# Order of the second network's first projection and the first network's third pair, and of two ScalarE steps

## The chip, the cores and the metric

The kernel runs on one core of a Trainium2 chip. The metric is the device time of one execution in microseconds. Its five engines run streams of their own: TensorE (PE; its weight loads are shown apart as PEld), VectorE (DVE), ScalarE (ACT), GpSimd (POOL) and SyncE (SP), which starts the DMA transfers here. They meet only through semaphores.

## The reference, cut to what matters

```python
kv_pool = kv.reshape(B, H // 4, 4, W // 4, 4, C).mean(axis=(2, 4))
k = v = kv_pool.reshape(B, -1, C) @ w_sr             # 768 keys, C = 128
s = (q @ k.transpose(0, 2, 1)) / np.sqrt(C)          # 12288 tokens
a = np.exp(s - s.max(-1, keepdims=True))
a /= a.sum(-1, keepdims=True) + 1e-09
x = (a @ v).reshape(-1, C)
h = x @ w_in                                         # first network, 128 -> 2048
x = (h * (1.0 / (1.0 + np.exp(-1.702 * h)))) @ w_out # 2048 -> 128
h = x @ w_in2                                        # second network
return (h * np.clip(h + 3.0, 0.0, 6.0) / 6.0) @ w_out2
```

## The kernel before, in words

The 12288 tokens are worked through in NT = 24 tiles of 512. Everything that TensorE multiplies is split into a high part (rounded to the format fp32r) and a low part (what is left), and each product is three matmuls: high by high, low weights by high data, high weights by low data. `product` (L1080 on) issues them, so nearly all matmuls of the profile have the lines L1082, L1083 and L1086.

A network's 2048 hidden features are handled as 8 pairs of 128-feature chunks (PAIRS = 8). For pair p of tile t:

- `hidden1(t, p)` and `hidden2(t, p)` (TensorE, 6 matmuls of 512 columns) compute the pair's hidden values of the first and the second network into PSUM. In the loop hidden1 always uses the tile pair[2], and waits for the gelu before it (`act1_ready`); hidden2 uses pair[0] and pair[1] in turn.
- First network: `gelu` (ScalarE, L589) takes PSUM to `work`, `act1_hi` (ScalarE, L604) rounds it to `mid_hi`, `act1_lo` (VectorE, L891) subtracts to `mid_lo`.
- Second network: `gate` (ScalarE, L616), `hard_swish` (VectorE, L904), `act2_hi` (ScalarE, L628) and `act2_lo` (VectorE, L912) do the same.
- `project1(t, p)` and `project2(t, p)` (TensorE, 6 matmuls each) multiply by the output weights and add up over the pairs in the PSUM banks `bank_av` and `bank_out`.

One loop turn i works on four tiles at once: the first network of tile i, the second network of tile i - 1, the attention scores of tile i + 2 and the weighing of values of tile i + 1. The order of every engine is written out by hand; there is no planner. Turn 1 has an order of its own, turns 2 to 21 are a hardware loop, turns 22 and 23 are written out with the same function and leave out the attention work for which no tile is left.

On TensorE, `job(i, j)` is hidden1(i, j/2) for even j and hidden2(i - 1, j/2 rounded down) for odd j; `finish_job(i, j)` is project1(i, ·) or project2(i - 1, ·) in the same way. A turn begins hidden2(i - 1, 0), hidden1(i, 0), project2(i - 2, 7), hidden2(i - 1, 1), hidden1(i, 1), project1(i, 0). Then j runs on from 4, each step followed by the projection three steps behind it (LAG = 3): hidden1(i, 2), project2(i - 1, 0), hidden2(i - 1, 2), project1(i, 1), and so on. After the last comes `between`: the scores for tile i + 2 and the weighing for tile i + 1.

The accumulator `bank_out` is used by one tile after another. So `project2` with p = 0 waits until the previous tile's result has been transposed out of it (`turn_y`, VectorE, L929, 128x512 to `y_sb`):

```python
pe.wait_ge(mid2_hi_ready, PAIRS * t + p + 1)      # L1383
if p == 0 and later(t) and output2_in(t) is bank_out:
    pe.wait_ge(y_ready, t)
```

At the start of a turn VectorE does, in this order: `scale_x` (L853), the inverse of the sums, `x1_low` (L862), the transposition of one tile's probabilities in four slots (`turn_p`, L836), of which the first three stand ahead of hard_swish 0 and the fourth behind it, then act1_lo 0, act2_lo 0, turn_y, hard_swish 1, act1_lo 1, `turn_q` (L804), act2_lo 1, act1_lo 2, hard_swish 2. ScalarE does gate 0, gelu 0, act1_hi 0, act2_hi 0, gelu 1, gate 1, act1_hi 1, gelu 2, act2_hi 1, act1_hi 2, gate 2, and then for each further pair gelu, act2_hi of the pair before, act1_hi, gate. An engine's instructions start strictly in order, so one that waits holds all behind it.

Of the kernel before, what the change touches and what calls it, by code (L numbers as in the profile page):

```python
# [12 lines left out]
def attention_and_two_ffns(nc, q, kv, w_sr, w_in1, w_out1, w_in2, w_out2, out):  # L13
# [17 lines left out]
    PAIRS = FC // 2  # L31
# [21 lines left out]
    with ExitStack() as ctx:  # L53
# [69 lines left out]
        def mid2(t, p):  # L123
            return (p + 2) % 4 if isinstance(t, int) and t == NT - 1 else 2 + p % 2
# [60 lines left out]
        def hidden1_in(t, p):  # L185
            return pair[(2, 1, 0)[p % 3]] if isinstance(t, int) and t == 0 else pair[2]
# [5 lines left out]
        def activated1(t, p):  # L192

            return hidden1_in(t, p)[:, :] if isinstance(t, int) and t == 0 else act1[p % 2]
# [115 lines left out]
        def of_pair(c):  # L310
            return slice(0, PAIR) if c is None else slice(c * TILE, (c + 1) * TILE)
# [4 lines left out]
        def in_pair(data, t, p, c):  # L316

            if c is not None and isinstance(t, int) and t == NT - 1 and p == PAIRS - 1:
                return data[:, :].rearrange("p (c n) -> p c n", c=2)[:, :, of_tile(c)]
            return data[:, of_pair(c)]  # L320
# [7 lines left out]
        def later(value):  # L328
            return not isinstance(value, int) or value > 0
# [173 lines left out]
        def _(act):  # L503
# [16 lines left out]
            def q_high(u):  # L520
                act.wait_ge(qt_ready, u - 1)
                if isinstance(u, int) and u == 2:
                    act.wait_ge(scores_ready, SLOTS)
                else:
                    act.wait_ge(scores_ready, SLOTS * u)
                act.activation(q_hi[:, :], q_t[:, :], ACT.Copy, scale=SCALE).then_inc(q_hi_ready, 1)
# [21 lines left out]
            def p_hi(t, n):  # L548
                act.wait_ge(p_landed, 16 * 16 * t)
                cols = slice(n * PAIR, (n + 1) * PAIR)  # L550
                act.activation(p_high[:, cols], p_keys[:, cols], ACT.Copy).then_inc(p_hi_ready, 1)
# [28 lines left out]
            def gelu(t, p, c=None):  # L580
                n = PAIRS * t + p
                part = of_pair(c)
                if c == 0:
                    act.wait_ge(h1_half_ready, 1)
                else:
                    act.wait_ge(h1_ready, n + 1)
                if later(t):
                    act.wait_ge(mid1_ready, n - 1)
                act.activation(activated1(t, p)[:, part], hidden1_in(t, p)[:, part],  # L589
                               ACT.Gelu_apprx_sigmoid).then_inc(act1_half_ready if c == 0 else act1_ready, 1)  # L590

            def act1_hi(t, p, c=None):
                n = PAIRS * t + p
                part = of_pair(c)
                if c == 0 and p == 0:
                    act.wait_ge(act1_half_ready, 1)
                else:
                    act.wait_ge(act1_ready, n + 1)
                if isinstance(t, int) and t == 0:
                    if p > 3:  # L600
                        act.wait_ge(out1_done, p - 3)
                else:
                    act.wait_ge(out1_done, n - 1)
                act.activation(mid_hi[mid1(t, p)][:, part], activated1(t, p)[:, part],  # L604
                               ACT.Copy).then_inc(mid1_half_hi_ready if c == 0 else mid1_hi_ready, 1)

            def gate(t, p, c=None):
                n = PAIRS * t + p
                first_half = p == 0 and c == 0
                if first_half:  # L610
                    act.wait_ge(h2_half_ready, 1)
                else:
                    act.wait_ge(h2_ready, n + 1 + (c if c and p else 0))
                if later(n - 1) and not c:
                    act.wait_ge(act2_ready, n - 1)
                act.activation(in_pair(gate2[p % 2], t, p, c), hidden_part(t, p, c), ACT.Relu,  # L616
                               bias=half[:, :], scale=1.0 / 6.0).then_inc(gate2_half_ready if first_half else gate2_ready, 1)

            def act2_hi(t, p, c=None):
                n = PAIRS * t + p  # L620
                act.wait_ge(act2_ready, n + 1 + (c or 0))
                if isinstance(t, int) and t == NT - 1 and p in (2, 3):
                    act.wait_ge(out1_done, PAIRS * NT)
                elif isinstance(t, int) and t == NT - 1 and p > 3:
                    act.wait_ge(out2_done, n - 3)
                elif later(n - 1):
                    act.wait_ge(out2_done, n - 1)
                act.activation(in_pair(mid_hi[mid2(t, p)], t, p, c), in_pair(act2[p % 2], t, p, c),  # L628
                               ACT.Copy).then_inc(mid2_hi_ready, 1)
# [7 lines left out]
            def load_table(func):  # L637
                act.activation(warm[:, :], half[:, :], func)
# [69 lines left out]
            def iteration(i, with_q=True, with_p=True, scored=True, begun=0, late=0):  # L708
                for p in range(begun, PAIRS):
                    if p == 0:  # L710
                        gate(i - 1, p)
                    if p == 1:
                        act2_hi(i - 1, p - 1)
                    gelu(i, p)
                    if p == 1:
                        gate(i - 1, p)
                    if 1 < p < PAIRS - 1:
                        act2_hi(i - 1, p - 1)
                    act1_hi(i, p)
                    if p == PAIRS - 1:  # L720
                        act2_hi(i - 1, p - 1)
                    if p > 1:
                        gate(i - 1, p)
                    if p == 3 + late and with_q:
                        q_high(i + 2)
                    if 4 + late <= p < 4 + late + P_PARTS and with_p:
                        p_hi(i + 1, p - 4 - late)
                if scored:
                    load_table(ACT.Exp)
                x2_high(i)  # L730
                act2_hi(i - 1, PAIRS - 1)
                if scored:
                    for s in range(SLOTS):
                        exponential(i + 2, s)
                if with_p:
                    x1_high(i + 1)
                if scored:
                    load_table(ACT.Gelu_apprx_sigmoid)

            iteration(1, begun=4, late=1)  # L740
            with act.Fori(2, NT - 2) as i:
                iteration(i)
# [336 lines left out]
        def _(pe):  # L1079
# [309 lines left out]
            def job(i, j):  # L1389
                if j % 2 == 0:  # L1390
                    hidden1(i, j // 2)
                else:
                    hidden2(i - 1, j // 2)

            def finish_job(i, j):
                if j % 2 == 0:
                    project1(i, j // 2)
                else:
                    project2(i - 1, j // 2)
# [49 lines left out]
            def iteration(i, scored_too=True, weighed=True):  # L1449

                if later(i - 1):
                    job(i, 1)
                    job(i, 0)
                    finish_job(i - 1, JOBS - 1)

                    job(i, 3)
                    job(i, 2)
                    finish_job(i, 0)
                    begun = 4
                else:  # L1460
                    hidden2(0, 0)
                    hidden2(0, 1)
                    hidden1(1, 0)
                    hidden2(0, 2)
                    hidden2(0, 3)
                    project2(0, 0)
                    hidden1(1, 1)
                    project1(1, 0)
                    hidden1(1, 2)
                    project2(0, 1)  # L1470
                    project1(1, 1)
                    hidden1(1, 3)
                    project1(1, 2)

                    project2(0, 2)
                    hidden1(1, 4)
                    begun = 9
                for j in range(begun, JOBS):
                    job(i, j)
                    if j >= LAG:  # L1480
                        finish_job(i, j - LAG)
                finish_job(i, JOBS - 2)
                if scored_too:
                    between(i)
                elif weighed:
                    for k in range(KC):
                        weigh(i + 1, k)
                finish_job(i, JOBS - 3)
# [38 lines left out]
```

## Time and profile before

| | us |
|---|---|
| median of three runs | 1280.79 (1280.19 to 1281.34) |
| the profiled execution's own time | 1280.32 |
| its span in the profile | 1278.6 |
| TensorE busy | 1270.0 (5800 matmuls) |
| VectorE busy | 1034.1 |
| ScalarE busy | 1027.4 |
| GpSimd busy | 34.4 |

The span runs from the first to the last instruction that the profiler saw; the time of the execution has 1.7 us more around it. Busy shares tell which engine could be the bound, the view of waits who stood still for whom, and a timeline of a short window in which order things end. In a timeline row the first number is the start and the second the duration. A matmul's duration overlaps its successor's, so a rate is read from the distances between starts. A weight load of an undelayed matmul starts together with the matmul before it. The profile numbers lines by kernel.py.

### The profile page before, as it was taken

To read this page: it belongs to the slowest core of one execution; us is meant where nothing else is said; L and a number is where in the kernel's file an instruction comes from. 1 tells how busy PE (TensorE), PEld (TensorE's weight loads), DVE (VectorE), ACT (ScalarE), POOL (GpSimd) and SP (SyncE) were. 2 spreads that over 40 slices of the span, in tenths; PEclk is the share of its full clock that TensorE was granted. 3 is DMA by queue.
4 is the path that set the end of the run, shared out by engine and by line. 5 is a ranking of instruction groups with operands and counts; after the bars stand their busy time and mean duration, and the time that the engine had idled before them with its cause. 6 is when DMAs were issued, how large, how long until landed. Compare 5 with 4: busy or idle time off the path is not lost.

```text
span 1278.6 us, 18310 instructions
## 1 busy us (share of the span) xinstructions
PE 1270.0 (99%) x5800; PEld 1055.4 (83%) x5800; DVE 1034.1 (81%) x1084; ACT 1027.4 (80%) x1216; POOL 34.4 (3%) x46
## 2 busy tenths in 40 slices
PE   8999999999999999999999999999999999999998
PEld 7888888888888888888888888888888888888887
DVE  5788887888878878888788888887888878887768
ACT  3888877888788888887788878888888778887776
POOL 1800000000000000000000000000000000000000
PEclk9999999999999999999999999999999999999999
DMA  8421321303213123032130220311303213022001
GB/s 280 126 44 40 75 46 28 74 9 65 57 17 74 30 44 74 0 74 49 25 74 13 60 63 11 74 34 40 74 0 74 49 25 74 18 47 67 1 9 17
DMA packets 183685, 65.69 MB, mean 51 GB/s; under 512 B 104560, under 2 KB 176368, under 8 KB 183408
## 3 DMA queue, kind: packets, MB, share of 16 engines
q1 hardware_dynamic: 182576, 65.30, 22.3%
q10 hardware_dynamic: 1088, 0.13, 0.1%
q8 instruction: 11, 0.18, 0.1%
q14 instruction: 10, 0.08, 0.0%
HBM read 22.87 MB, written 6.34 MB: 23 GB/s over the span
## 4 chain that ended last, share of the span: by engine, by line
PE 97%; SPq 1%; DMA 1%; DVE 0%; ACT 0%; issue 0%; DVEq 0%
PE pair L1082 14%; PE pair L1083 14%; PE pair L1086 14%; PE bank_av L1082 9%; PE bank_av L1083 9%; PE bank_av L1086 9%; PE bank_out L1086 7%; PE bank_out L1083 7%; PE bank_out L1082 7%; PE score_banks L1086 2%; PE score_banks L1083 2%; PE score_banks L1082 2%; DMA kv_sb<-in_kv_dram 1%; SPq L354 0%; SPq L362 0%; SPq L366 0%
## 5 line engine op out<-in xcount | busy, mean ns | idle before, releaser
L912 DVE TENSOR_TENSOR mid_lo<-work,mid_hi 128x1024 fp32r<-128x1024 f32 (+1 forms) x193 | 233.9, 1212 | 112.5 <-ACT mid_hi L628 112.4
L1082 PE MATMUL pair<-x_hi,w_hi 128*128 128x512 f32 (+1 forms) x774 | 300.7, 388 | 0.0
L1083 PE MATMUL pair<-x_hi,w_lo 128*128 128x512 f32 (+1 forms) x774 | 300.0, 388 | 0.0
L1086 PE MATMUL pair<-x_lo,w_hi 128*128 128x512 f32 (+1 forms) x774 | 299.9, 387 | 0.0
L589 ACT ACTIVATE work<-pair 128x1024 f32<-128x1024 f32 x184 | 189.2, 1028 | 120.8 <-PE pair L1086 118.5
L904 DVE SCALAR_TENSOR_TENSOR work<-work,pair 128x1024 f32<-128x1024 f32 (+1 forms) x194 | 232.9, 1201 | 15.3 <-ACT work L616 14.6
L891 DVE TENSOR_TENSOR mid_lo<-work,mid_hi 128x1024 fp32r<-128x1024 f32 x184 | 223.6, 1215 | 25.1 <-ACT mid_hi L604 25.0
L616 ACT ACTIVATE work<-pair,half 128x1024 f32<-128x1024 f32 (+1 forms) x194 | 213.1, 1099 | 4.3 <-PE pair L1086 4.2
L628 ACT ACTIVATE mid_hi<-work 128x1024 fp32r<-128x1024 f32 (+1 forms) x193 | 201.8, 1046 | 2.3 <-DVE work L904 2.3
L604 ACT ACTIVATE mid_hi<-work 128x1024 fp32r<-128x1024 f32 x184 | 194.7, 1058 | 1.6
L1082 PEld LDWEIGHTS pair<-x_hi,w_hi 128*128 128x128 f32 x774 | 145.3, 188 | 33.7 <-ACT work L589 4.2
L1086 PEld LDWEIGHTS pair<-x_lo,w_hi 128*128 128x128 f32 x774 | 145.4, 188 | 29.8
L1083 PEld LDWEIGHTS pair<-x_hi,w_lo 128*128 128x128 f32 x774 | 145.4, 188 | 28.8
L1086 PE MATMUL bank_av<-mid_lo,w_hi 128*128 128x512 f32 x398 | 154.9, 389 | 0.0
L1082 PE MATMUL bank_av<-mid_hi,w_hi 128*128 128x512 f32 x398 | 154.9, 389 | 0.0
L1083 PE MATMUL bank_av<-mid_hi,w_lo 128*128 128x512 f32 x398 | 154.8, 389 | 0.0
L1086 PE MATMUL bank_out<-mid_lo,w_hi 128*128 128x512 f32 x368 | 143.2, 389 | 0.0
L1082 PE MATMUL bank_out<-mid_hi,w_hi 128*128 128x512 f32 x368 | 143.2, 389 | 0.0
L1083 PE MATMUL bank_out<-mid_hi,w_lo 128*128 128x512 f32 x368 | 143.2, 389 | 0.0
L541 ACT ACTIVATE probs<-score_banks,neg_max 128x768 f32<-128x768 f32 x88 | 78.1, 900 | 80.8 <-DVE neg_max L813 80.8
L813 DVE TENSOR_REDUCE neg_max<-score_banks 128x1 f32<-128x768 f32 x88 | 78.3, 950 | 42.6 <-PE score_banks L1086 42.6
L1086 PEld LDWEIGHTS bank_av<-mid_lo,w_hi 128*128 128x128 f32 x398 | 74.7, 188 | 15.7 <-DVE mid_lo L891 0.2
(175 smaller groups left out, 1560.2 us busy)
## 6 DMA issues: line engine op xcount, KB each, us to landing
p_keys<-p_turned SPq DMA_DIRECT2D x368, 96.0 KB, 2.2
inv_b<-inv_dram SPq DMA_DIRECT2D x23, 256.0 KB, 3.2
out_dram<-y_sb SPq DMA_DIRECT2D x92, 64.0 KB, 2.4
q_raw<-in_q_dram SPq DMA_DIRECT2D x88, 64.0 KB, 2.0
kv_sb<-in_kv_dram SPq DMA_DIRECT2D x6, 768.0 KB, 9.4
w_raw<-in_moe_w_in_dram SPq DMA_DIRECT2D x2, 1024.0 KB, 8.0
kv_sb<-in_kv_dram SPq DMA_DIRECT2D x6, 256.0 KB, 8.1
inv_dram<-inv_t SPq DMA_DIRECT2D x92, 0.5 KB
```

The source lines that it names most:

```text
L541: act.activation(two(slot(dst, s)), scored_slot(u, s), ACT.Exp, bias=neg_max[:, s:s + 1], accum_out=p_sum[:, s:s + 1]).then_inc(exp_ready, 1)
L589: act.activation(activated1(t, p)[:, part], hidden1_in(t, p)[:, part], ACT.Gelu_apprx_sigmoid).then_inc(act1_half_ready if c == 0 else act ...
L604: act.activation(mid_hi[mid1(t, p)][:, part], activated1(t, p)[:, part], ACT.Copy).then_inc(mid1_half_hi_ready if c == 0 else mid1_hi_read ...
L616: act.activation(in_pair(gate2[p % 2], t, p, c), hidden_part(t, p, c), ACT.Relu, bias=half[:, :], scale=1.0 / 6.0).then_inc(gate2_half_rea ...
L628: act.activation(in_pair(mid_hi[mid2(t, p)], t, p, c), in_pair(act2[p % 2], t, p, c), ACT.Copy).then_inc(mid2_hi_ready, 1)
L813: dve.reduce_max(neg_max[:, s:s + 1], scored_slot(u, s), AX_XY, negate=True).then_inc(max_ready, 1)
L891: dve.tensor_tensor(mid_lo[mid1(t, p)][:, part], activated1(t, p)[:, part], mid_hi[mid1(t, p)][:, part], ALU.subtract).then_inc(mid1_half_ ...
L904: last = dve.scalar_tensor_tensor(out=in_pair(act2[p % 2], t, p, c), in0=in_pair(gate2[p % 2], t, p, c), scalar=1.0, in1=hidden_part(t, p, c),
L912: dve.tensor_tensor(in_pair(mid_lo[mid2(t, p)], t, p, c), in_pair(act2[p % 2], t, p, c), in_pair(mid_hi[mid2(t, p)], t, p, c), ALU.subtrac ...
L1082: pe.matmul(dst, a_hi, b_hi, start=start, stop=False)
L1083: pe.matmul(dst, a_lo, b_hi, start=False, stop=False)
L1086: return pe.matmul(dst, a_hi, b_lo, start=False, stop=stop)
```

## The change

On TensorE, in turns 2 to 23, project2(i - 1, 0) is issued ahead of hidden1(i, 2) instead of behind it: the turn begins hidden2 0, hidden1 0, project2(i - 2, 7), hidden2 1, hidden1 1, project1 0, project2 0, hidden1 2, and then goes on as before with hidden2 2, project1 1. On ScalarE, in the same turns, act2_hi 1 is issued ahead of gelu 2 instead of behind it. Turn 1, whose pairs below 4 are written out apart on ScalarE, isn't touched. The number of instructions, their shapes, the buffers and the conditions they wait for are the same.

```diff
--- before.py
+++ after.py
@@ -711,10 +711,12 @@
                         gate(i - 1, p)
                     if p == 1:
                         act2_hi(i - 1, p - 1)
+                    if p == 2:
+                        act2_hi(i - 1, p - 1)
                     gelu(i, p)
                     if p == 1:
                         gate(i - 1, p)
-                    if 1 < p < PAIRS - 1:
+                    if 2 < p < PAIRS - 1:
                         act2_hi(i - 1, p - 1)
                     act1_hi(i, p)
                     if p == PAIRS - 1:
@@ -1456,7 +1458,9 @@
                     job(i, 3)
                     job(i, 2)
                     finish_job(i, 0)
-                    begun = 4
+                    finish_job(i, 1)
+                    job(i, 4)
+                    begun = 5
                 else:
                     hidden2(0, 0)
                     hidden2(0, 1)
```

## Rows read from the trace of the kernel before

**Rows 1.** The page: TensorE busy, and its granted clock in slices.
```profile
PE 1270.0 (99%) x5800; PEld 1055.4 (83%) x5800; DVE 1034.1 (81%) x1084; ACT 1027.4 (80%) x1216; POOL 34.4 (3%) x46
...
PEclk9999999999999999999999999999999999999999
```

**Rows 2.** Waits; who waited for whom: us in total, times, longest us.
```profile
PEld pair L1082 <- ACT work L589: 4.2, 23, 0.2
```

**Rows 3.** Busy time of each engine in two windows (x instructions).
```profile
532.90:584.72 51.82, 51.82 (x236) 43.03 (x235) 42.54 (x45) 42.59 (x50) 0.00 (x0) 1.00 0.21 46
...
588.72:598.27 9.55, 9.55 (x44) 7.81 (x43) 9.34 (x13) 8.30 (x11) 0.00 (x0) 1.00 0.11 25
```

**Rows 4.** Timeline, TensorE, turn 11: start, duration in us, [idle before <- releaser].
```profile
597.42 0.39 PE L1083 MATMUL bank_av<-mid_hi,w_lo 128*128 128x512 f32 x1
...
597.65 0.39 PE L1086 MATMUL bank_av<-mid_lo,w_hi 128*128 128x512 f32 x1
597.79 0.19 PEld L1082 LDWEIGHTS pair<-x_hi,w_hi 128*128 128x128 f32 x1 [0.18 <-ACT work L589]
...
599.29 0.39 PE L1082 MATMUL bank_out<-mid_hi,w_hi 128*128 128x512 f32 x1
```

**Rows 5.** Timeline, VectorE, the same turn, and the instructions of line 929.
```profile
588.72 0.69 DVE L853 TENSOR_TENSOR x_full<-bank_av,inv_b 128x512 f32<-128x512 f32 x1 [0.30 <-PE bank_av L1086]
...
596.43 1.21 DVE L912 TENSOR_TENSOR mid_lo<-work,mid_hi 128x1024 fp32r<-128x1024 f32 x1
597.56 0.71 DVE L929 STREAM_TRANSPOSE y_sb<-bank_out 128x512 f32<-128x512 f32 x1
598.78 1.22 DVE L904 SCALAR_TENSOR_TENSOR work<-work,pair 128x1024 f32<-128x1024 f32 x1 [0.51 <-ACT work L616]
...
L929 DVE STREAM_TRANSPOSE y_sb<-bank_out x23: 708/711/718, 131.0 to 1253.9; 128x512 f32<-128x512 f32 x23
```

**Rows 6.** Timeline, ScalarE, the same turn.
```profile
594.74 1.04 ACT L628 ACTIVATE mid_hi<-work 128x1024 fp32r<-128x1024 f32 x1
596.71 1.03 ACT L589 ACTIVATE work<-pair 128x1024 f32<-128x1024 f32 x1 [0.93 <-PE pair L1086]
...
599.58 1.02 ACT L589 ACTIVATE work<-pair 128x1024 f32<-128x1024 f32 x1
...
604.93 1.03 ACT L589 ACTIVATE work<-pair 128x1024 f32<-128x1024 f32 x1 [1.43 <-PE pair L1086]
```

**Rows 7.** Timeline, turn 2 and turn 23.
```profile
131.02 0.71 DVE L929 STREAM_TRANSPOSE y_sb<-bank_out 128x512 f32<-128x512 f32 x1
...
131.27 0.39 PE L1086 MATMUL bank_av<-mid_lo,w_hi 128*128 128x512 f32 x1
...
1214.74 0.71 DVE L929 STREAM_TRANSPOSE y_sb<-bank_out 128x512 f32<-128x512 f32 x1
...
1215.33 0.39 PE L1086 MATMUL bank_av<-mid_lo,w_hi 128*128 128x512 f32 x1
...
1215.81 0.40 PE L1083 MATMUL pair<-x_hi,w_lo 128*128 128x512 f32 x1
```

**Rows 8.** Timeline, before the loop: a load behind VectorE.
```profile
20.30 0.68 DVE L798 SCALAR_TENSOR_TENSOR q_lo<-bank_out,q_hi 128x512 fp32r<-128x512 f32 x1
...
21.10 0.19 PEld L1082 LDWEIGHTS pair<-k_hi,q_hi 128*128 128x128 f32 x1
```

**Rows 9.** Timeline, before the loop: a late load and the matmuls around it.
```profile
73.63 0.39 PE L1086 MATMUL pair<-x_lo,w_hi 128*128 128x512 f32 x1
...
73.98 0.19 PEld L1082 LDWEIGHTS pair<-x_hi,w_hi 128*128 128x128 f32 x1 [0.39 <-ACT probs L541]
...
75.96 0.39 PE L1086 MATMUL pair<-x_lo,w_hi 128*128 128x512 f32 x1
```

**Rows 10.** Timeline, TensorE, the first microseconds: eight like matmuls, twice.
```profile
2.92 4.18 PE L1170 MATMUL pair<-patch,ident 128*128 128x288 f32 x8 [2.92 <-POOL ident L463]
...
8.62 2.14 PE L1170 MATMUL pair<-patch,ident 128*128 128x288 f32 x8
```

## The prediction

> **What bounds the kernel now.** I read the page's busy shares first. TensorE is busy 1270.0 of 1278.6 us, at the full granted clock (2.4 GHz of its two levels) in all 40 slices [rows 1]. So the time is TensorE's instruction stream plus whatever holds it up, and any new gap in that stream is paid in full.
>
> Next comes the view of waits, kept to TensorE's weight loads, since that is where a stalled matmul shows. One wait belongs to the loop: 23 times, 0.2 us at most, 4.2 us in all, on ScalarE's gelu, L589 [rows 2]. Then the busy times in a window of one loop turn: 51.82 us long, TensorE busy for all of it, while VectorE and ScalarE work 42.5 us each [rows 3]. With so little to take away, I went to the timeline of the place that the diff touches, first TensorE [rows 4], then VectorE [rows 5] and ScalarE [rows 6].
>
> **What can be gained.** hidden1(i, 2) must wait until gelu 1 has emptied the one PSUM pair that all of hidden1 uses. gelu 1 runs from 596.71 to 597.74 [rows 6]. The weight load follows at 597.79, where an undelayed one starts together with the matmul before it, at 597.65 [rows 4]. That is 0.14 us late, but loads run ahead of matmuls, so little of it is lost. The undelayed distance between 128x512 matmuls is 0.227 us (597.42 to 597.65). From 597.65 to 599.29 lie seven of them, 1.59 us undelayed, and they took 1.64. So the turn loses 0.05 us; turn 23 loses 0.04 (1215.33 to 1215.81, two distances, 0.48 against 0.45 at least; the rest follows) [rows 7]. The change sends six matmuls, project2(i - 1, 0), ahead, 6 x 0.227 = 1.36 us, and gelu 1 is then done long before. The wait goes in the 22 turns i = 2 to 23 that take the changed branch: 22 x 0.04 = 0.9 us. The 23rd is in turn 1, whose order is written out apart and stays. This is all that there is to gain, 0.07%.
>
> **What the moved step meets.** project2(i - 1, 0) issues six matmuls and no DMA, but it has three conditions: the high half of pair 0, its low half, and y_ready at L1384, because it opens a new sum in bank_out and VectorE must first have transposed the previous tile's result out of that bank (turn_y, L929). Today it starts at 599.29, when all three are met. Moved, its first weight load is due at 597.65 and its first matmul 0.227 after that. The high half is ready: rounding ends at 594.74 + 1.04 = 595.78 [rows 6]. The low half ends at 596.43 + 1.21 = 597.64, and the third matmul, whose load is due near 598.10, needs it; no loss. But turn_y runs from 597.56 to 598.27 [rows 5]. It is 0.62 us too late for a load due at 597.65.
>
> Could VectorE be earlier? Its work there hangs on TensorE itself: scale_x starts at 588.72 after an idle 0.30 that ends with TensorE's weighing, and in the 9.55 us from there to the end of turn_y VectorE is busy 9.34 us in 13 instructions [rows 3, 5]. Nothing that TensorE does in between is reordered before project1(i, 0) ends, and VectorE's order is untouched. So the 0.62 us stays in every turn and cannot heal by itself: if TensorE stalls, the next turn's scores come later and VectorE's chain with them.
>
> **The cost of one stall.** The load starts some time after turn_y ends. Lower bound 0.05 us, as after gelu 1 (597.74 to 597.79) [rows 4, 6]. Upper bound 0.12, from a place where TensorE also stands behind several waits in line: q_lo ends at 20.98, the load starts at 21.10 [rows 8]. The delay of the load is thus 0.67 to 0.74; since project2 has two waits ahead of its first matmul, I take 0.72. Not all of the load's delay is lost. At 73.98 a load came 0.35 us after its due time 73.63; from 73.63 to 75.96 lie nine distances, 2.04 undelayed, and they took 2.33: 0.29 lost, 0.06 less than the delay [rows 9]. At 597.79 it was 0.09 less. So a stall costs 0.58 to 0.68; I take 0.64.
>
> It isn't the same in all turns. Turn_y stands 23 times in the trace, of 708 to 718 ns [rows 5]; turns 3 to 22, twenty of them, look like the one shown. In turn 2 it ends at 131.73 against a due time of 131.27, 0.46 late: 0.46 + 0.10 - 0.08 = 0.48. In turn 23 no probabilities are turned any more; it ends at 1215.45 against 1215.33: 0.12 + 0.10 - 0.08 = 0.14 [rows 7].
>
> **What else moves.** Behind the waiting matmul stand, in TensorE's strict order, hidden1(i, 2), hidden2(i - 1, 2) and project1(i, 1). hidden1(i, 2) now starts 1.36 + 0.64 = 2.0 us later than before and gelu 2, which started at 599.58 with its input just complete, can't start before about 601.4. Here ScalarE's reordering matters: act2_hi 1 waits for hard_swish 1, which ends at 598.78 + 1.22 = 600.00 [rows 5], so it runs 600.05 to 601.10 in time that ScalarE would now idle, and gelu 2 follows at 601.4 undelayed, ending at 602.4. hidden1(i, 3) has its load due at about 603.7 (project2, hidden1, hidden2 and project1, 24 matmuls or 5.44 us, after 598.5, less one distance), 1.3 us of slack. The edit of ScalarE's order costs nothing; were gelu 2 left ahead of it, act2_hi 1 would start near 602.3, and it too is only needed by project2(i - 1, 1) some 3 us later. From pair 3 on the order is the old one, and ScalarE waits for TensorE there (1.43 us before the gelu at 604.93 [rows 6]), so nothing else becomes late. No DMA queue is passed.
>
> **The sum.** Against the profiled execution's own 1280.32 us (span 1278.6, 1.7 around it): 20 x 0.64 = 12.8, + 0.48 + 0.14 = 13.4, - 0.9 regained = + 12.5, so 1292.8. That execution lay 0.5 us below the median 1280.79 of the runs shown; with half of that I predict 1293.0 us, slower by 0.95%. By the bounds, 20 x 0.58 + 0.6 - 0.9 = + 11.3 and 20 x 0.68 + 0.6 - 0.9 = + 13.3.
>
> **Rivals.**
> Rival A, the wait is hidden (not slower). Mechanism: turn_y's end falls before the load's due time, so only the old stall goes: 1280.8 - 0.9 = 1279.9. It decides from the point at which VectorE's stretch from 588.72 to 598.27 is 0.62 us shorter. Turn 23 speaks for it, where the transposes of probabilities are gone; the lateness is 0.12 [rows 7]; but twenty turns carry them, and nothing in the change removes any. A gain over 0.2%, 2.6 us, would need three times the whole loss that exists.
>
> Rival B, a second wait: gelu 2, behind act2_hi 1, becomes late for hidden1(i, 3). The 1.3 us of slack would have to be used up; a further 0.3 us a turn gives 1293 + 22 x 0.3 = 1299.6. The idle rows of ScalarE speak against it.
>
> Rival C, the clock: a gap in each turn makes TensorE fall to the lower of its levels for a while. The first eight 288-column matmuls of the trace took 4.18 us, eight later ones 2.14 [rows 10], so a matmul may double. If only the twelve after the gap did, 12 x 0.227 = 2.7 us a turn, 22 x 2.7 = 60 us, 1353. Against it: after the 0.39 us gap at 73.98 the distances were back at 0.227 within five matmuls [rows 9]. The clock row shows no dip in any slice [rows 1], but it reads 9 in the first slice too, which holds the slow eight, so the distances are the better witness. The Trainium skill, "TensorE: Matmul & The Clock Gate", section "A second HAM failure mode: psum-queue depth-cycling", says that small gaps between matmul groups, one per cycle of a PSUM queue, can make the clock swing; by that rule rival C holds, and the trace so far disagrees, with gaps half as long.
>
> **Chances.** Forecast 0.90, A 0.04, B 0.03, C 0.01; the last 0.02 for a gain by something that I don't see. About 0.2% is what a measurement of this kernel can tell from no change. So slower 0.94, same 0.04, faster 0.02. The range holds the forecast with its bounds (1291.6 to 1294.1 by the runs' median), widened for the spread of runs and a mis-sized restart to 1290.0 to 1295.5.
>
> **What would show it.** Right: in the waits, the gelu entry shrinks from 23 to one or two, and a new one, bank_out's weight loads behind VectorE's L929, stands some 22 times with 0.6 to 0.7 us each, about 14 us. A turn is 52.4 instead of 51.82 us. Wrong: no idle before bank_out in turn 3 to 22 (rival A), idle before pair's loads behind L589 later in the turn (B), or distances of 0.4 us after the gap (C). The forecast falls if turn_y isn't what releases project2, or if its end is earlier against TensorE than 0.6 us after the due time.

## The result, and the profile after

The changed kernel takes 1292.57 us (median of five runs, 1292.35 to 1293.27) against 1280.79: ratio 1.0094, 95% interval 1.0083 to 1.0106. The forecast was 1293.0 us, with a range of 1290.0 to 1295.5. The profiled execution took 1292.57 us, its span 1290.8. In kernel.py the lines behind the ScalarE edit stand two further down: L1082, L1083 and L1086 are now L1084, L1085 and L1088, L912 is L914, turn_y's L929 is L931.

The page first, busy times and granted clock. The clock is as in [rows 1]. The number of matmuls is the same, and the weight loads' busy time too (1055.0 us against 1055.4). "PE busy" rose by 4 us, not by 12: the modelled duration of a matmul overlaps its successor's and covers a part of each gap.

```profile
PE 1274.1 (99%) x5800; PEld 1055.0 (82%) x5800; DVE 1036.2 (80%) x1084; ACT 1035.4 (80%) x1216; POOL 34.5 (3%) x46
...
PEclk9999999999999999999999999999999999999999
```

The waits. Of the 23 waits on the gelu in [rows 2] one is left, that of turn 1; new are 22 loads of bank_out that stood idle for 16.3 us in all. Of each idle (0.77 us in most turns), some 0.04 us are the ordinary space between two loads, so the delay is 0.73.

```profile
PEld bank_out L1084 <- issue: 16.3, 22, 0.8
...
PE bank_out L1084 <- DVE y_sb L931: 7.7, 21, 0.4
...
PEld pair L1084 <- ACT work L589: 0.2, 1, 0.2
```

These two rows are the same event. The load's row says "issue" and the matmul's row names turn_y, with less than half of the time. The wait for y_ready is an instruction of its own in TensorE's queue ahead of the load, so nothing on the load itself names a releaser. The views leave this instruction out, but the trace holds it: in turn 11 a semaphore instruction of L1386 stands from 603.34 to 603.39, just ahead of the load at 603.41.

A loop turn (columns as in [rows 3]: length, then PE, PEld, DVE, ACT busy). It is 52.42 us long, 0.60 more than in [rows 3], and for 0.38 us of it TensorE isn't busy.

```profile
551.18:603.60 52.42, 52.04 (x235) 43.01 (x235) 42.63 (x44) 42.94 (x51) 0.00 (x0) 1.00 0.21 45
```

The place of the change in turn 11, as in [rows 4] and [rows 5]: start, duration, and idle with its releaser.

```profile
602.45 0.39 PE L1085 MATMUL bank_av<-mid_hi,w_lo 128*128 128x512 f32 x1
...
602.59 0.71 DVE L931 STREAM_TRANSPOSE y_sb<-bank_out 128x512 f32<-128x512 f32 x1
...
602.68 0.39 PE L1088 MATMUL bank_av<-mid_lo,w_hi 128*128 128x512 f32 x1
603.41 0.19 PEld L1084 LDWEIGHTS bank_out<-mid_hi,w_hi 128*128 128x128 f32 x1 [0.77 <-issue]
603.45 0.47 PE L1084 MATMUL bank_out<-mid_hi,w_hi 128*128 128x512 f32 x1 [0.38 <-DVE y_sb L931]
...
603.75 0.40 PE L1085 MATMUL bank_out<-mid_hi,w_lo 128*128 128x512 f32 x1
...
604.22 0.40 PE L1084 MATMUL bank_out<-mid_hi,w_hi 128*128 128x512 f32 x1
```

The last matmul of project1(i, 0) starts at 602.68, and bank_out's first load is due with it. turn_y ends at 602.59 + 0.71 = 603.30 and the load starts at 603.41. From 602.68 to 604.22 lie four distances (the matmul between 603.75 and 604.22 isn't shown), 0.91 us undelayed, and they took 1.54: 0.63 lost. The turns say the same: 51.82 us before, with 0.04 lost to the gelu, and 52.42 now, so the stall costs 0.60 + 0.04 = 0.64 us.

Turn 2 and turn 23, in answer to [rows 7]: loads due at 131.03 and 1227.45 start at 131.60 and 1227.69.

```profile
130.78 0.71 DVE L931 STREAM_TRANSPOSE y_sb<-bank_out 128x512 f32<-128x512 f32 x1
...
131.03 0.39 PE L1088 MATMUL bank_av<-mid_lo,w_hi 128*128 128x512 f32 x1
131.60 0.19 PEld L1084 LDWEIGHTS bank_out<-mid_hi,w_hi 128*128 128x128 f32 x1 [0.60 <-issue]
...
1226.86 0.71 DVE L931 STREAM_TRANSPOSE y_sb<-bank_out 128x512 f32<-128x512 f32 x1
...
1227.45 0.39 PE L1088 MATMUL bank_av<-mid_lo,w_hi 128*128 128x512 f32 x1
...
1227.69 0.19 PEld L1084 LDWEIGHTS bank_out<-mid_hi,w_hi 128*128 128x128 f32 x1 [0.28 <-issue]
```

ScalarE after the gap: act2_hi 1 ends at 606.12, gelu 2 waits for TensorE until 606.47.

```profile
605.06 1.06 ACT L628 ACTIVATE mid_hi<-work 128x1024 fp32r<-128x1024 f32 x1 [0.34 <-DVE work L906]
606.47 1.03 ACT L589 ACTIVATE work<-pair 128x1024 f32<-128x1024 f32 x1 [0.34 <-PE pair L1088]
```

### The profile page after: what moved, and what is told of

It is laid out like the page before. It is cut to its first block, busy times and chain, and to the rows that moved or that the text cites. A ratio compares the mean times of both kernels' runs of the same rounds, so it can differ in the third digit from the quotient of the medians.

```text
span 1290.8 us, 18310 instructions
## 1 busy us (share of the span) xinstructions
PE 1274.1 (99%) x5800; PEld 1055.0 (82%) x5800; DVE 1036.2 (80%) x1084; ACT 1035.4 (80%) x1216; POOL 34.5 (3%) x46
## 4 chain that ended last, share of the span: by engine, by line
PE 82%; DVE 11%; issue 4%; ACT 1%; DVEq 1%; DMA 1%; SPq 0%
PE pair L1084 11%; PE pair L1088 11%; PE pair L1085 11%; PE bank_av L1088 9%; PE bank_av L1084 9%; PE bank_av L1085 9%; PE bank_out L1084 5%; PE bank_out L1088 5%; PE bank_out L1085 5%; DVE p_turned L838 3%; PE score_banks L1088 2%; PE score_banks L1085 2%; PE score_banks L1084 2%; DVE mid_lo L914 2%; DVE work L906 2%
## 5 line engine op out<-in xcount | busy, mean ns | idle before, releaser
L914 DVE TENSOR_TENSOR mid_lo<-work,mid_hi 128x1024 fp32r<-128x1024 f32 (+1 forms) x193 | 233.8, 1212 | 106.8 <-ACT mid_hi L628 106.7
L1084 PE MATMUL pair<-x_hi,w_hi 128*128 128x512 f32 (+1 forms) x774 | 300.2, 388 | 0.0
L1088 PE MATMUL pair<-x_lo,w_hi 128*128 128x512 f32 (+1 forms) x774 | 299.9, 387 | 0.0
L1085 PE MATMUL pair<-x_hi,w_lo 128*128 128x512 f32 (+1 forms) x774 | 299.8, 387 | 0.0
L628 ACT ACTIVATE mid_hi<-work 128x1024 fp32r<-128x1024 f32 (+1 forms) x193 | 201.6, 1045 | 9.8 <-DVE work L906 9.8
L1084 PEld LDWEIGHTS pair<-x_hi,w_hi 128*128 128x128 f32 x774 | 145.3, 188 | 30.4 <-ACT probs L541 0.4
L1088 PEld LDWEIGHTS pair<-x_lo,w_hi 128*128 128x128 f32 x774 | 145.4, 188 | 29.8
L1085 PEld LDWEIGHTS pair<-x_hi,w_lo 128*128 128x128 f32 x774 | 145.3, 188 | 29.7
L1088 PE MATMUL bank_av<-mid_lo,w_hi 128*128 128x512 f32 x398 | 154.9, 389 | 0.0
L1084 PE MATMUL bank_av<-mid_hi,w_hi 128*128 128x512 f32 x398 | 154.9, 389 | 0.0
L1085 PE MATMUL bank_av<-mid_hi,w_lo 128*128 128x512 f32 x398 | 154.9, 389 | 0.0
L1084 PE MATMUL bank_out<-mid_hi,w_hi 128*128 128x512 f32 x368 | 145.0, 394 | 7.7 <-DVE y_sb L931 7.7
L1088 PE MATMUL bank_out<-mid_lo,w_hi 128*128 128x512 f32 x368 | 143.3, 389 | 0.0
L1085 PE MATMUL bank_out<-mid_hi,w_lo 128*128 128x512 f32 x368 | 143.3, 389 | 0.0
L1084 PEld LDWEIGHTS bank_out<-mid_hi,w_hi 128*128 128x128 f32 x368 | 69.0, 188 | 29.8 <-issue 16.3
```

The lines of the kernel that those rows point to most:

```text
L914: dve.tensor_tensor(in_pair(mid_lo[mid2(t, p)], t, p, c), in_pair(act2[p % 2], t, p, c), in_pair(mid_hi[mid2(t, p)], t, p, c), ALU.subtrac ...
L1084: pe.matmul(dst, a_hi, b_hi, start=start, stop=False)
L1085: pe.matmul(dst, a_lo, b_hi, start=False, stop=False)
L1088: return pe.matmul(dst, a_hi, b_lo, start=False, stop=stop)
```

## The experiments

All times are medians of 4 to 11 runs; the kernel before took 1280.5 to 1280.7 us beside them. "Ratio" is against the kernel before, with its 95% interval.

### ScalarE's half alone

```diff
 # against the changed kernel, TensorE
-                    finish_job(i, 1)
-                    job(i, 4)
-                    begun = 5
+                    begun = 4
```

> Only ScalarE's half of the change: act2_hi 1 ahead of gelu 2, TensorE in the old order. My theory: ScalarE's order costs nothing. act2_hi 1 starts when hard_swish 1 has ended (600.00 in the trace of before), gelu 2 follows at 601.1 instead of 599.6 and ends at 602.1, a microsecond ahead of the load of hidden1(i, 3), due at 603.15. So 1280.8 us, within 0.3 of before. Rival (part of the loss comes from ScalarE): if gelu 2 became late for hidden1(i, 3), this kernel would be slower than before, by up to the whole 11.8 us.

Measured: 1280.74 us, ratio 0.9999 (0.9990 to 1.0008). The gelu's entry in the waits is that of before, and in the timeline gelu 2 follows act2_hi 1 (548.74, L628) at 549.71 and ends at 550.71, 1.13 us ahead of the load of hidden1(i, 3) at 551.84. The waits:

```profile
PEld pair L1084 <- ACT work L589: 4.2, 23, 0.2
```

The timeline of ScalarE in turn 10:

```profile
548.74 1.06 ACT L628 ACTIVATE mid_hi<-work 128x1024 fp32r<-128x1024 f32 x1 [0.34 <-DVE work L906]
549.71 1.00 ACT L589 ACTIVATE work<-pair 128x1024 f32<-128x1024 f32 x1
```

ScalarE's edit has no part in the loss.

### TensorE's half alone

```diff
 # against the changed kernel, ScalarE
-                    if p == 2:
-                        act2_hi(i - 1, p - 1)
                     gelu(i, p)
...
-                    if 2 < p < PAIRS - 1:
+                    if 1 < p < PAIRS - 1:
                         act2_hi(i - 1, p - 1)
```

> Only TensorE's half: project2(i - 1, 0) ahead of hidden1(i, 2), ScalarE in the old order with gelu 2 ahead of act2_hi 1. My theory: the whole loss is here, 1292.6 us, within 0.3 of the changed kernel, with the same 0.77 us idle ahead of bank_out's first weight load in every turn. Rival: if the rounding step ahead of gelu 2 were what costs, this kernel would be back near 1280; if on the contrary it saved something, this one would be slower than 1292.6.

Measured: 1292.86 us, ratio 1.0094 (1.0079 to 1.0110), with the changed kernel's two rows of waits to the tenth. ScalarE now idles 1.72 us before gelu 2 and rounds pair 1 behind it. VectorE's act2_lo 1 waits for that, 1.66 us in the turn shown, but no load of TensorE gets a new wait from it. The whole loss is in TensorE's order. The waits:

```profile
PEld bank_out L1082 <- issue: 16.3, 22, 0.8
...
PE bank_out L1082 <- DVE y_sb L929: 7.7, 21, 0.4
```

The timeline of ScalarE and VectorE in turn 10:

```profile
555.07 1.03 ACT L589 ACTIVATE work<-pair 128x1024 f32<-128x1024 f32 x1 [1.72 <-PE pair L1086]
555.99 1.05 ACT L628 ACTIVATE mid_hi<-work 128x1024 fp32r<-128x1024 f32 x1
...
557.07 1.23 DVE L912 TENSOR_TENSOR mid_lo<-work,mid_hi 128x1024 fp32r<-128x1024 f32 x1 [1.66 <-ACT mid_hi L628]
```

### turn_y made early: both waits gone

```diff
 # against the changed kernel, VectorE
-                    if p == 0 and with_p:
-                        turn_p(i + 1, 3)
                     if p == 1:
                         hard_swish(i - 1, p)
...
                     if p == 0:
-                        act2_lo(i - 1, p)
                         turn_y(i - 2)
+                        act2_lo(i - 1, p)
+                    if p == 0 and with_p:
+                        turn_p(i + 1, 3)
```

> The changed kernel, and VectorE's turn_y moved up: the fourth turn_p of a turn goes from ahead of act1_lo 0 to behind act2_lo 0, and turn_y goes ahead of act2_lo 0. My theory (the wait on turn_y is all of the loss): act1_lo 0 then runs 594.9 to 596.1 on the old scale, turn_y 596.0 to 596.7, act2_lo 0 to 597.85; loads due at 597.65 and 598.10, so neither wait is late, nor is gelu 1's. Expected 1279.9 us, 0.9 under before. Rival (any reordering of project2 and hidden1 costs some 0.6 us a turn by itself, through the PSUM banks or the weight loads): stays near 1292.6. Rival (turn_p is too late for the transfers of the probabilities behind it): a new wait of ScalarE or TensorE on the weighing, 1285 or more.

Measured: 1279.40 us (eleven runs, 1279.15 to 1279.79), ratio 0.9990 (0.9981 to 0.9999). This is the fastest kernel of the study. In the rows: a turn is 51.78 us with TensorE busy throughout; turn_y ends at 544.94, 0.94 ahead of the load due at 545.88; act2_lo 0 ends at 546.05, and the loads follow each other at 0.227 us. turn_p (L838) now fills the place in which VectorE used to idle before hard_swish 1 (0.51 us in [rows 5]). The busy times in one turn:

```profile
532.57:584.35 51.78, 51.78 (x236) 43.10 (x235) 42.71 (x45) 42.82 (x50) 0.00 (x0) 1.00 0.21 46
```

The timeline of VectorE in turn 10:

```profile
544.23 0.71 DVE L931 STREAM_TRANSPOSE y_sb<-bank_out 128x512 f32<-128x512 f32 x1
544.87 1.18 DVE L914 TENSOR_TENSOR mid_lo<-work,mid_hi 128x1024 fp32r<-128x1024 f32 x1
545.97 0.97 DVE L838 STREAM_TRANSPOSE p_turned<-probs 128x768 f32<-128x768 f32 x1
547.00 1.22 DVE L906 SCALAR_TENSOR_TENSOR work<-work,pair 128x1024 f32<-128x1024 f32 x1
```

And of TensorE's weight loads:

```profile
545.88 0.19 PEld L1084 LDWEIGHTS bank_out<-mid_hi,w_hi 128*128 128x128 f32 x1
546.10 0.19 PEld L1085 LDWEIGHTS bank_out<-mid_hi,w_lo 128*128 128x128 f32 x1
546.33 0.19 PEld L1088 LDWEIGHTS bank_out<-mid_lo,w_hi 128*128 128x128 f32 x1
```

So moving project2(i - 1, 0) costs nothing by itself, and it wins back what the gelu's stall had cost, once the bank is free in time. By the times the gain is 1.3 us, and the interval leaves 0.1 to 2.4; the rows show 0.04 us a turn, 0.9 in 22. The rival of a fixed price per reordering falls, and so does that of late probabilities.

### VectorE's order alone, with TensorE as before

The same VectorE edit, on the kernel before.

> The kernel before, with VectorE's order of the experiment beside it (fourth turn_p behind act2_lo 0, turn_y ahead of act2_lo 0) and nothing else. My theory: VectorE's order is no gain in itself, since TensorE's only stall in the old order is gelu 1: 1280.8 us, within 0.3 of before, with the 0.18 us idle on L589 in 23 turns as before. Rival (VectorE's order helps TensorE by itself, for instance by sooner low halves): as fast as the experiment beside it, 1279.9 or less.

Measured: 1280.74 us, ratio 1.0002 (0.9993 to 1.0011). The gelu's wait stands as before:

```profile
PEld pair L1082 <- ACT work L589: 4.2, 23, 0.2
```

VectorE's order is worth nothing without the moved projection; the 1.3 us between this kernel and the one above, measured side by side, need both edits.

### How late turn_y is: a smaller lateness

```diff
 # against the changed kernel, VectorE
-                    if p == 0 and with_p:
-                        turn_p(i + 1, 3)
...
                     if p == 0:
                         act2_lo(i - 1, p)
                         turn_y(i - 2)
+                    if p == 0 and with_p:
+                        turn_p(i + 1, 3)
```

> The changed kernel, and on VectorE only the fourth turn_p of a turn moved from ahead of act1_lo 0 to behind turn_y. act1_lo 0 can't move up by the whole 0.88 us, since it needs act1_hi 0 (ends 594.83 on the old scale); turn_y then ends about 597.86 instead of 598.27. My theory (the loss is the lateness of turn_y's end, one for one): the load comes 0.32 us late instead of 0.73, a stall costs 0.24 instead of 0.64, 20 turns x 0.24 + 0.2 for turns 2 and 23 - 0.9 = + 4.1, so 1284.9 us. Rival (the loss is a fixed price of the moved step): 1292.6.

Measured: 1284.40 us, ratio 1.0030 (1.0019 to 1.0042). The load is 548.45 - 548.12 = 0.33 us late, as worked out. The waits:

```profile
PEld bank_out L1084 <- issue: 7.7, 22, 0.4
```

The timeline of turn 10:

```profile
547.62 0.71 DVE L931 STREAM_TRANSPOSE y_sb<-bank_out 128x512 f32<-128x512 f32 x1
...
548.12 0.39 PE L1088 MATMUL bank_av<-mid_lo,w_hi 128*128 128x512 f32 x1
...
548.45 0.19 PEld L1084 LDWEIGHTS bank_out<-mid_hi,w_hi 128*128 128x128 f32 x1 [0.36 <-issue]
```

### turn_y first: the next condition in line

```diff
 # against the changed kernel, VectorE
                     if p == 0:
-                        act2_lo(i - 1, p)
                         turn_y(i - 2)
+                        act2_lo(i - 1, p)
```

> The changed kernel, and on VectorE only turn_y and act2_lo 0 change places. turn_y ends at 597.14 on the old scale, in time; act2_lo 0 ends at 598.27, and the third matmul of project2(i - 1, 0), whose load is due at 598.10, needs it. My theory: the wait moves there, with a load 0.22 us late, some 0.13 lost a turn: 20 x 0.13 - 0.9 = + 1.7, so 1282.5 us, and the idle stands ahead of bank_out's load of line L1088 on VectorE's L914. Rival (project2's first matmul is held by something else than turn_y): 1292.6.

Measured: 1281.39 us, ratio 1.0007 (0.9997 to 1.0016), 1.1 less than expected. The wait moved to where it was expected, the third matmul's load (L1088) behind act2_lo 0 (L914), 21 times; the load is 546.64 - 546.45 = 0.19 us late. I had put 0.22: act2_lo 0 takes 1.18 us here, not 1.21. Against the kernel with neither wait, 2.0 us over 21 turns are 0.09 a turn instead of the 0.13 that I had allowed. The waits:

```profile
PEld bank_out L1088 <- DVE mid_lo L914: 4.7, 21, 0.2
```

The timeline of turn 10:

```profile
545.40 1.18 DVE L914 TENSOR_TENSOR mid_lo<-work,mid_hi 128x1024 fp32r<-128x1024 f32 x1
...
546.45 0.39 PE L1085 MATMUL bank_out<-mid_hi,w_lo 128*128 128x512 f32 x1
546.64 0.19 PEld L1088 LDWEIGHTS bank_out<-mid_lo,w_hi 128*128 128x128 f32 x1 [0.23 <-DVE mid_lo L914]
...
546.98 0.40 PE L1084 MATMUL bank_out<-mid_hi,w_hi 128*128 128x512 f32 x1
```

### A larger lateness

```diff
 # against the changed kernel, TensorE
-                    finish_job(i, 0)
                     finish_job(i, 1)
+                    finish_job(i, 0)
                     job(i, 4)
```

> The changed kernel, and project2(i - 1, 0) goes one step further up, ahead of project1(i, 0) too. VectorE's order is the changed kernel's. Its load is now due 1.36 us sooner while turn_y ends where it did. My theory: the stall grows by the whole step, to 0.64 + 1.36 = 2.0 us in turns 3 to 22, 1.86 in turn 2 and 1.5 in turn 23: + 43.5 - 0.9 = + 42.6, so 1323 us, the distance of matmuls outside the gaps staying at 0.227. Rival (a stall of fixed size, whatever the position): 1292.6. Rival (longer gaps bring TensorE to its lower clock): distances near 0.45 behind the gaps and well over 1330.

Measured: 1323.24 us, ratio 1.0332 (1.0315 to 1.0350). The load is due at 560.20 and starts at 562.30, 2.10 us late. Behind the gap the first distance is 0.30 us (562.33 to 562.63), and from the second on they are 0.23 to 0.24, so TensorE came out of it at the upper of its two levels; the granted clock from 562.30 to 566.00 is 1.00. The waits:

```profile
PEld bank_out L1084 <- issue: 46.2, 22, 2.1
```

The timeline of turn 10:

```profile
560.20 0.39 PE L1088 MATMUL pair<-x_lo,w_hi 128*128 128x512 f32 x1
...
561.47 0.71 DVE L931 STREAM_TRANSPOSE y_sb<-bank_out 128x512 f32<-128x512 f32 x1
...
562.30 0.19 PEld L1084 LDWEIGHTS bank_out<-mid_hi,w_hi 128*128 128x128 f32 x1 [2.13 <-issue]
...
562.33 0.47 PE L1084 MATMUL bank_out<-mid_hi,w_hi 128*128 128x512 f32 x1 [1.74 <-DVE y_sb L931]
...
562.63 0.39 PE L1085 MATMUL bank_out<-mid_hi,w_lo 128*128 128x512 f32 x1
...
562.87 0.40 PE L1088 MATMUL bank_out<-mid_lo,w_hi 128*128 128x512 f32 x1
...
563.10 0.40 PE L1084 MATMUL bank_out<-mid_hi,w_hi 128*128 128x512 f32 x1
```

### One wait instead of two

```diff
 # against the changed kernel, TensorE, in project2
-                pe.wait_ge(mid2_hi_ready, PAIRS * t + p + 1)
                 if p == 0 and later(t) and output2_in(t) is bank_out:
                     pe.wait_ge(y_ready, t)
+                else:
+                    pe.wait_ge(mid2_hi_ready, PAIRS * t + p + 1)
```

> The changed kernel, with one wait in place of two ahead of project2(i - 1, 0): it waits for y_ready alone. (The rounded halves of pair 0 are written before turn_y in VectorE's own order, so what it computes is the same.) In the changed kernel the load starts 0.11 us after turn_y ends, where a load behind one wait started 0.05 after gelu 1. My theory: the difference is the wait that stands as an instruction of its own ahead of the load; with one wait the load starts 0.05 us after turn_y's end, each of the 22 stalls is 0.06 shorter, 1.3 us in all, so 1291.3 us. Rival (the 0.11 us belong to VectorE's transposition, whose result is later to be seen than its row ends): 1292.6, with the load still 0.11 us behind.

Measured: 1291.96 us, ratio 1.0091 (1.0074 to 1.0108). The load starts at 550.93, 0.05 us behind turn_y's end at 550.88, so the 0.06 us more in the changed kernel belong to the second wait, not to the transposition. What they are worth was overestimated: 0.6 us less than the changed kernel, where 1.3 was expected. The intervals are too wide to tell the one from the other by the times, but the rows side with the smaller: from turn 3 to turn 22 the load starts at 184.16 and at 1179.53, so nineteen turns of 52.39 us, where the changed kernel has 184.05 and 1179.94, turns of 52.42. A turn is thus 0.03 us shorter with the load 0.06 sooner; why the other half isn't gained stays open. Note that the view of waits now names turn_y on the load itself. The waits:

```profile
PEld bank_out L1084 <- DVE y_sb L931: 14.9, 22, 0.7
```

The timeline of turn 10:

```profile
550.17 0.71 DVE L931 STREAM_TRANSPOSE y_sb<-bank_out 128x512 f32<-128x512 f32 x1
...
550.26 0.39 PE L1088 MATMUL bank_av<-mid_lo,w_hi 128*128 128x512 f32 x1
550.93 0.19 PEld L1084 LDWEIGHTS bank_out<-mid_hi,w_hi 128*128 128x128 f32 x1 [0.71 <-DVE y_sb L931]
```

## Why the prediction was right

The lateness of one load orders the six kernels that have it. Delay of the load in turns 3 to 22, from the rows above and, for TensorE's half alone, from its trace, against the time over the kernel without stalls (1279.4 us). The times come from several sets of runs, in which the kernel before took 1280.5 to 1280.8:

| kernel | load late, us | waits in the view | time, us | over 1279.4 |
|---|---|---|---|---|
| turn_y made early | none | 0 | 1279.40 | |
| turn_y first | 0.19 | 21 | 1281.39 | 2.0 |
| fourth turn_p late | 0.33 | 22 | 1284.40 | 5.0 |
| one wait | 0.67 | 22 | 1291.96 | 12.6 |
| changed kernel | 0.73 | 22 | 1292.57 | 13.2 |
| TensorE's half alone | 0.73 | 22 | 1292.86 | 13.5 |
| one step further up | 2.10 | 22 | 1323.24 | 43.8 |

From the third row to the last the load gets later by 1.77 us and the kernel longer by 38.8 us, 1.76 for each of 22 turns: what is added to the lateness is lost one for one. Each stall as such costs about 0.1 us less than the load is late: 0.33 us late in 22 turns would be some 7 us, and the time grew by 5.0.

By its own steps:

- **What can be gained**, 0.9 us: right by the rows. It can't be seen in the changed kernel, but in the one without either wait, whose turn is 51.78 us, 0.04 less than in [rows 3]; the times, 1.3 us with a wide interval, neither confirm nor contradict it. The two distances named for turn 23 give 0.03, not the 0.04 that was used.
- **What the moved step meets**: right, with both halves of pair 0 in time and turn_y 0.62 us late, the same 0.62 after as before (603.30 to 602.68). That VectorE's chain stays fixed to TensorE's, and the stall thus comes back in each turn, held: the load is 0.73 or 0.74 us late in every one of turns 3 to 22.
- **The cost of one stall**: a load delayed by 0.72, of which 0.64 is lost. Measured 0.73 and 0.64. For the time from turn_y's end to the load, the upper bound from [rows 8] was the right neighbour, for the reason given, as the kernel with one wait shows.
- **Turns 2 and 23**: the loads are late by 0.57 and 0.24 us, in the forecast 0.56 and 0.22.
- **ScalarE's edit at nothing**: right, shown from both sides. gelu 2 started 0.34 us after act2_hi 1 had ended.
- **Rival A** (the wait is hidden) is false here, and names the right remedy: with the stretch of VectorE ahead of turn_y shortened, the kernel came to 1279.4 where 1279.9 was said. **Rival B** (a second wait behind gelu 2) did not occur. **Rival C** (the clock) is false for one gap of up to 2.1 us a turn: a first distance of 0.30 us, then 0.23 to 0.24. The Trainium skill, "TensorE: Matmul & The Clock Gate", section "A second HAM failure mode: psum-queue depth-cycling", says that small idles between groups of matmuls, where they come frequently enough, make the clock swing; with one a turn, these traces don't show it.
- **What would show it**: right in the count (22 for bank_out, one left for the gelu's kind) and in the turn's length. It was wrong in the name: I expected turn_y as the releaser of the loads, 14 us, and the view has 16.3 us of "issue".

The sum came out 0.4 us above the median. Half of that is the 0.2 added for the profiled run's place among the runs. The other half is too small to be told from the spread of the runs. In the inner bounds one slip stands: "1291.6 to 1294.1 by the runs' median" has its lower end from the profiled execution; by the median (1280.79 + 11.3) it is 1292.1. The stated range doesn't hang on it.

## What to carry to other kernels

When a step is moved up on the bound engine, write down every condition that it waits for, also the one that frees its accumulator, and compare each one's end with the new due time of the weight load that needs it. The one that is latest against its load sets the price; here it was paid once for each turn, because the chain behind it starts from the bound engine's own results and didn't catch up. When that one is mended, look at the next: with turn_y in time, act2_lo 0 was late. Moving VectorE's transposition ahead of work that had time to spare turned the same edit here from a loss of 0.9% into a gain of 0.1%. An entry "issue" in the waits of weight loads may be a wait that stands as an instruction of its own.

## What the runs showed of the hardware

- In these traces the load behind two waits started 0.11 us after the releaser's end (603.30 to 603.41), the one behind a single wait 0.05 (550.88 to 550.93).
- Where a weight load came 0.19 to 2.1 us late, TensorE lost about 0.1 us less than that (0.73 late, 0.64 lost).
- Gaps of 0.4 to 2.1 us, once in a turn of 52 to 54 us in which TensorE otherwise worked without a break, left it at the upper level of its clock (distances of 0.23 us behind them).
